# One transpose for the lower columns of two token blocks, and copies within SBUF that double the rows

## What is computed

```python
# mix: w is softmaxed over k, 8 heads of 24 columns share a weight
out = np.einsum('bshk,bskhg->bshg', w, x_unf)
# gated product
gate = 1.0 / (1.0 + np.exp(-(x @ w_gate)))          # 192 -> 1536
y = (gate * (x @ w_val)) @ w_out                    # 1536 -> 192
# rational product
h = y @ w_in                                        # 192 -> 2048
P = a[0] + a[1]*h + a[2]*h**2 + a[3]*h**3
Q = 1.0 + abs(b[0])*abs(h) + abs(b[1])*h**2
z = (P / (Q + 1e-06)) @ w_out2                      # 2048 -> 192
```

## Time and profile before

| | |
|---|---|
| median of 3 runs | 1420.21 us (1420.18 to 1420.8) |
| the profiled execution | 1422.31 us, its span 1420.4 us |
| mean granted clock of PE | 0.993 of full |
| busy share of the span: PE, PEld | 97%, 87% |
| DVE, ACT, POOL | 89%, 76%, 25% |
| mean share of the 16 DMA engines on the SP queue | 7.2% |

### The profile page before, as it was taken

The page is one execution under the profiler, slowest core; times in us unless marked ns, Lnnn a source line. Parts: engine busy times, 40 slices in busy tenths (PEclk is TensorE's granted clock), DMA queues, the critical chain, the costliest instruction groups (busy, mean ns, idle before and its releaser), DMA issues.

```text
span 1420.4 us, 19056 instructions
## 1 busy us (share of the span) xinstructions
PE 1379.2 (97%) x7282; PEld 1238.5 (87%) x7282; DVE 1259.2 (89%) x1504; ACT 1083.4 (76%) x1470; POOL 356.2 (25%) x204
## 2 busy tenths in 40 slices
PE   6899999999999999999999999999999999999976
PEld 5789888888889889889889889889898898889966
DVE  7677989999989989889999989899898898889998
ACT  3387887877777788787787777787787778778975
POOL 0143323231332313233131332323233141210000
PEclk9999999999999999999999999999999999999989
DMA  9100100101010010100101010010100001000000
GB/s 242 59 32 1 38 0 1 42 1 43 1 43 1 1 43 1 43 1 0 43 1 43 0 43 1 0 43 0 42 1 29 11 1 34 1 12 0 12 0 17
DMA packets 13468, 33.06 MB, mean 23 GB/s; under 512 B 1601, under 2 KB 7747, under 8 KB 13377
## 3 DMA queue, kind: packets, MB, share of 16 engines
q1 hardware_dynamic: 13312, 31.85, 7.2%
q0 software_dynamic: 64, 0.00, 0.0%
HBM read 25.55 MB, written 6.29 MB: 22 GB/s over the span
## 4 chain that ended last, share of the span: by engine, by line
PE 90%; DVE 6%; ACT 2%; issue 2%; DMA 0%; SPq 0%; DVEq 0%
PE ring L319 49%; PE acc L346 39%; PE ring L373 1%; PE ring L376 1%; DVE work L712 1%; DVE work L719 1%; DVE work L733 1%; DVE work L706 1%; DVE u L700 1%; DVE work L742 0%; DVE work L726 0%; DVE work L653 0%; DMA window<-in_x_dram 0%; ACT work L485 0%; ACT work L487 0%
## 5 line engine op out<-in xcount | busy, mean ns | idle before, releaser
L346 PE MATMUL acc<-out_w,work 128*128 128x192 f32 x2048 | 366.3, 330 | 14.6 <-DVE work L742 14.6
L346 PEld LDWEIGHTS acc<-out_w,work 128*128 128x128 f32 x2048 | 342.5, 193 | 21.4 <-DVE work L742 15.0
L484 ACT ACTIVATE work<-ring,coef 128x512 f32<-128x512 f32 (+1 forms) x272 | 182.2, 670 | 223.9 <-PE ring L319 221.4
L319 PE MATMUL ring<-yt,in_w 128*128 128x512 f32 (+1 forms) x1360 | 330.8, 389 | 2.4 <-DVE work L712 1.9
L346 PE MATMUL acc<-out_w,u 128*128 128x192 f32 x1536 | 284.8, 327 | 6.3 <-DVE u L700 6.3
L319 PEld LDWEIGHTS ring<-yt,in_w 128*128 128x128 f32 x1360 | 245.7, 189 | 51.4 <-DVE work L712 2.9
L319 PE MATMUL ring<-xt,gate_w 128*128 128x512 f32 (+1 forms) x1020 | 267.5, 392 | 3.4 <-DVE work L712 2.1
L346 PEld LDWEIGHTS acc<-out_w,u 128*128 128x128 f32 x1536 | 256.7, 190 | 13.5 <-DVE u L700 7.2
L319 PE MATMUL ring<-xt,val_w 128*128 128x512 f32 (+1 forms) x1020 | 257.0, 382 | 0.0
L603 POOL TENSOR_TENSOR mixed<-mixed,prod 128x768 f32<-128x768 f32 (+1 forms) x90 | 196.7, 2186 | 169.9 <-DVE u L700 150.7
L598 POOL TENSOR_TENSOR prod<-window,mixw 128x768 f32<-128x768 f32 (+1 forms) x90 | 135.0, 1500 | 408.3 <-DVE work L719 307.1
(11 more groups left out here) (57 smaller groups left out, 921.1 us busy)
## 6 DMA issues: line engine op xcount, KB each, us to landing
window<-in_x_dram SPq DMA_DIRECT2D x14, 960.0 KB, 4.6
out_dram<-zsb SPq DMA_DIRECT2D x15, 384.0 KB, 2.5
out_w<-in_moe_w_out_dram SPq DMA_DIRECT2D x1, 1536.0 KB, 19.1
mixw<-in_weight_gen_dram SPq DMA_DIRECT2D x13, 112.0 KB, 2.9
out_w<-in_moe_w_out_dram SPq DMA_DIRECT2D x2, 576.0 KB, 8.7
work<-in_moe_w_in_dram SPq DMA_DIRECT2D x2, 512.0 KB
work<-in_moe_w_in_dram SPq DMA_DIRECT2D x4, 256.0 KB, 13.4
window<-in_x_dram SPq DMA_DIRECT2D x1, 768.0 KB, 4.3
```

What stands on the lines that cost most here:

```text
L319: last = nc.tensor.matmul(dst, wt[:, c], xs[:, 0:n], start=at == 0, stop=at == 4)
L346: last = nc.tensor.matmul(dst, src[:, n * P:(n + 1) * P], w[:, i, :], start=i == 0 and n % 2 == 0, stop=i == last_i and n % 2 == 1, skip_g ...
L484: nc.scalar.activation(den(n), h, ACT.Abs, scale=coef[:, 6:7])
```

## The change

For x tiles from the third on and for all y tiles, the lower columns of two neighbouring token blocks stand side by side in one block of 128 columns (`x_side`, `y_side`), and one transpose turns both: the rows 0 to 63 that come out belong to the first block, rows 64 to 127 to the second. ACT and DVE split this half-as-wide bank into `xs[0]`, `xs[1]` (or `ys`), and SP issues copies from SBUF to SBUF that put each half of the rows into both halves of `xt[..][2]` and `[3]` (or `yt`): four transfers for the high part as soon as ACT has written it, four for the low part when DVE has. PE's first product of the tile waits for all eight. `x_twice` is left for the first two tiles only; POOL writes the last add of a mix in two instructions, the second straight into `x_side`.

```diff
+            def spread(part, n, dst, signal):
+                for h in range(2):
+                    src = part[h * DB:(h + 1) * DB, 0:n * P // 2].rearrange("p (a t) -> p a t", t=P)
+                    for d in range(2):
+                        to = dst[d * DB:(d + 1) * DB, 0:n * P].rearrange("p (a h t) -> p a h t", h=2, t=P)
+                        sp.dma_start(to[:, :, h, :].bitcast(F32), src.bitcast(F32)).then_inc(signal, 16)
+            def spread_x(j):
+                sp.wait_ge(s_xh, 2 * j + 2)
+                spread(xs[0], BLOCKS[j], xt[j % 2][2], s_xs)
+                sp.wait_ge(s_x, 2 * j + 2)
+                spread(xs[1], BLOCKS[j], xt[j % 2][3], s_xs)
...
             for c in range(EARLY, NCH):
                 if c + 1 < NCH:
                     load_weights(c + 1)
+                if c >= 3:
+                    spread_y(c - 3)
                 load_window(c)
                 if c >= 4:
                     store(c - 4)
+                if c > EARLY:
+                    spread_x(c - 1)
...
                 if i == 0:
                     pe.wait_ge(s_x, 2 * j + 2)
+                    wait(pe, s_xs, 128 * (j - EARLY + 1))
...
                 if i == 0:
                     pe.wait_ge(s_y, 2 * j + 2)
+                    pe.wait_ge(s_ys, 128 * (j + 1))
...
-                for n in range(BLOCKS[j]):
+                for n in range(count):
                     last = nc.tensor.transpose(bank(u, j, 1)[:, n * P:(n + 1) * P], lower(n), ident[:, :])
...
+                    pe.wait_ge(s_mix, MIXES * (j - EARLY + 1))
+                    transposes("X", j, lambda n: mixed[:, n, 0:DA],
+                               lambda n: x_side[:, n * P:(n + 1) * P], BLOCKS[j] // 2).then_inc(s_xT, 1)
...
+                nc.scalar.copy(xs[0][:, 0:n // 2], bank("X", j, 1)[:, 0:n // 2]).then_inc(s_xh, 1)
...
-                nc.scalar.copy(dst[:, :, :, 0:D], src)
-                nc.scalar.copy(dst[:, :, :, D:2 * P], src[:, :, :, DA:D]).then_inc(s_ysb, 1)
+                nc.scalar.copy(ysb[:, 0:n * DA].rearrange("p (a n d) -> p a n d", n=2, d=DA), src[:, :, :, 0:DA])
+                nc.scalar.copy(y_side[:, 0:n * DB].rearrange("p (a n d) -> p a n d", n=2, d=DB),
+                               src[:, :, :, DA:D]).then_inc(s_ysb, 1)
...
-                if k % 4 == 3 and k > 3:
-                    x_twice(k // 4 + 1)
...
+                if k == MIXES - 1:
+                    nc.gpsimd.tensor_tensor(mixed[:, 0:n, 0:DA], mixed[:, 0:n, 0:DA], prod[:, 0:n, 0:DA], ALU.add)
+                    nc.gpsimd.tensor_tensor(x_side[:, 0:n * DB].rearrange("p (n d) -> p n d", d=DB), mixed[:, 0:n, DA:D],
+                                            prod[:, 0:n, DA:D], ALU.add).then_inc(s_mix, 1)
+                    return
...
+                nc.vector.tensor_tensor(xs[1][:, 0:n // 2], bank("X", j, 1)[:, 0:n // 2],
+                                        xs[0][:, 0:n // 2].bitcast(F32), ALU.subtract).then_inc(s_x, 1)
```

More of the change, by code:

```diff
@@ L116, in moe_kernel @@
         yt = [[sb(f"yt{b}_{n}", [P, T], F32R) for n in range(4)] for b in range(2)]
-        x_pair = sb("x_pair", [P, J, 2, DB])
-        ysb = sb("ysb", [P, J, 2 * P])
+        xs = [sb(f"xs{n}", [P, T // 2], F32R) for n in range(2)]
+        ys = [sb(f"ys{n}", [P, T // 2], F32R) for n in range(2)]
+        x_side = sb("x_side", [P, J * 2 * DB])
+        ysb = sb("ysb", [P, J * DA])
+        y_side = sb("y_side", [P, J * DB])
         zsb = sb("zsb", [P, J, D])
@@ L191, in moe_kernel @@
         s_x = sem("x_ready")
+        s_xs = sem("x_lower_rows_spread")
         s_gate = sem("gate_done")
@@ L200, in moe_kernel @@
         s_y = sem("y_ready")
+        s_ys = sem("y_lower_rows_spread")
         s_h = sem("h_done")
@@ L282, in load_weights, with spread_y @@
                 sp.dma_start(weights(c), wg_rows[:, OFFS[c] * HK:OFFS[c + 1] * HK]).then_inc(s_weights[c % FIRST], 16)
+            def spread(part, n, dst, signal):
[9 more added lines that the diff above has]
+                spread(xs[1], BLOCKS[j], xt[j % 2][3], s_xs)
+            def spread_y(j):
+                sp.wait_ge(s_yh, 2 * j + 2)
+                spread(ys[0], BLOCKS[j], yt[j % 2][2], s_ys)
+                sp.wait_ge(s_y, 2 * j + 2)
+                spread(ys[1], BLOCKS[j], yt[j % 2][3], s_ys)
             def store(j):
@@ L308, in _ @@
                     store(c - 4)
-            for j in range(NCH - 4, NCH):
+                if c > EARLY:
+                    spread_x(c - 1)
+            spread_y(NCH - 3)
+            store(NCH - 4)
+            spread_x(NCH - 1)
+            spread_y(NCH - 2)
+            store(NCH - 3)
+            spread_y(NCH - 1)
+            for j in range(NCH - 2, NCH):
                 store(j)
@@ L367, in out2, with transposes @@
                 second_product(acc2, out2_w, num(n), i, F2 - 1, BLOCKS[j]).then_inc(s_out2, 1)
-            def transposes(u, j, upper, lower):
+            def transposes(u, j, upper, lower, count):
                 wait_bank(pe, u, j, 0)
@@ L379, in x_transposes @@
             def x_transposes(j):
-                pe.wait_ge(s_twice, j + 1)
-                transposes("X", j, lambda n: mixed[:, n, 0:DA],
-                           lambda n: x_pair[:, n, :, :].rearrange("p a d -> p (a d)")).then_inc(s_xT, 1)
+                if j < EARLY:
+                    pe.wait_ge(s_twice, j + 1)
+                    transposes("X", j, lambda n: mixed[:, n, 0:DA],
+                               lambda n: x_side[:, n * P:(n + 1) * P], BLOCKS[j]).then_inc(s_xT, 1)
+                else:
+                    pe.wait_ge(s_mix, MIXES * (j - EARLY + 1))
+                    transposes("X", j, lambda n: mixed[:, n, 0:DA],
+                               lambda n: x_side[:, n * P:(n + 1) * P], BLOCKS[j] // 2).then_inc(s_xT, 1)
             def y_transposes(j):
                 pe.wait_ge(s_ysb, j + 1)
-                transposes("Y", j, lambda n: ysb[:, n, 0:DA], lambda n: ysb[:, n, DA:2 * P]).then_inc(s_yT, 1)
+                transposes("Y", j, lambda n: ysb[:, n * P:(n + 1) * P], lambda n: y_side[:, n * P:(n + 1) * P],
+                            BLOCKS[j] // 2).then_inc(s_yT, 1)
             def keep_busy(count, m=0):
@@ L441, in x_twice @@
             def x_twice(j):
[L442 to L447, removed]
+                act.wait_ge(s_early, EARLY_STEPS * OFFS[j + 1])
                 wait(act, s_xT, j)
                 n = BLOCKS[j]
-                nc.scalar.copy(x_pair[:, 0:n, :, :], mixed[:, 0:n, DA:D].unsqueeze(2).to_broadcast([P, n, 2, DB])
+                nc.scalar.copy(x_side[:, 0:n * 2 * DB].rearrange("p (n a d) -> p n a d", a=2, d=DB), mixed[:, 0:n, DA:D].unsqueeze(2).to_broadcast([P, n, 2, DB])
                                ).then_inc(s_twice, 1)
@@ L459, in x_high @@
                 nc.scalar.copy(dst[0][:, 0:n], bank("X", j, 0)).then_inc(s_xh, 1)
-                nc.scalar.copy(dst[2][:, 0:n], bank("X", j, 1)).then_inc(s_xh, 1)
+                if j < EARLY:
+                    nc.scalar.copy(dst[2][:, 0:n], bank("X", j, 1)).then_inc(s_xh, 1)
+                    return
+                wait(act, s_xs, 128 * (j - EARLY))
+                nc.scalar.copy(xs[0][:, 0:n // 2], bank("X", j, 1)[:, 0:n // 2]).then_inc(s_xh, 1)
             def y_high(j):
@@ L468, in y_high @@
                 nc.scalar.copy(dst[0][:, 0:n], bank("Y", j, 0)).then_inc(s_yh, 1)
-                nc.scalar.copy(dst[2][:, 0:n], bank("Y", j, 1)).then_inc(s_yh, 1)
+                wait(act, s_ys, 128 * j)
+                nc.scalar.copy(ys[0][:, 0:n // 2], bank("Y", j, 1)[:, 0:n // 2]).then_inc(s_yh, 1)
             def sigmoid(m):
@@ L680, in x_low @@
                 dve.wait_ge(s_xh, 2 * j + 2)
-                nc.vector.tensor_tensor(dst[3][:, 0:n], bank("X", j, 1), dst[2][:, 0:n].bitcast(F32),
-                                        ALU.subtract).then_inc(s_x, 1)
+                if j < EARLY:
+                    nc.vector.tensor_tensor(dst[3][:, 0:n], bank("X", j, 1), dst[2][:, 0:n].bitcast(F32),
+                                            ALU.subtract).then_inc(s_x, 1)
+                    return
+                nc.vector.tensor_tensor(xs[1][:, 0:n // 2], bank("X", j, 1)[:, 0:n // 2],
+                                        xs[0][:, 0:n // 2].bitcast(F32), ALU.subtract).then_inc(s_x, 1)
             def y_low(j):
@@ L691, in y_low @@
                 dve.wait_ge(s_yh, 2 * j + 2)
-                nc.vector.tensor_tensor(dst[3][:, 0:n], bank("Y", j, 1), dst[2][:, 0:n].bitcast(F32),
-                                        ALU.subtract).then_inc(s_y, 1)
+                nc.vector.tensor_tensor(ys[1][:, 0:n // 2], bank("Y", j, 1)[:, 0:n // 2],
+                                        ys[0][:, 0:n // 2].bitcast(F32), ALU.subtract).then_inc(s_y, 1)
             def gated(m):
```

2 lines of the change are left out of this document (1 added, 1 removed).

## The result

The changed kernel takes 1412.99 us (median of 5 runs, 1410.86 to 1413.46) against 1420.8 us of the kernel before beside it (5 runs, 1420.18 to 1422.01): ratio 0.9942, 95% interval 0.9927 to 0.9956. The forecast was 1413.8 us in a range of 1411.2 to 1418.6. The profiled execution took 1412.99 us with a span of 1411.1 us.

The account below looks back on a forecast made before the run. PE, busy throughout 130 to 1320 us, was taken to bound the kernel. 59 transposes x 0.109 = 6.4 us, all else counted at nothing: 1420.2 - 6.4 = 1413.8 us, range 1411.2 to 1418.6 us.

Parts of the forecast that it names:

- What bounds the kernel: From 130 to 1320 us PE is busy 1190.00 of 1190.00 us; time off DVE or ACT gains nothing there.
- The price of a transpose: On PE, one lower transpose removed saves 0.109 us, the distance from start to start, not its 273 ns busy time.
- Rival D: On PE, each removed transpose gives back its busy time, 59 x 0.273 = 16.1 us, so 1404 us; chance 2%.
- 59 of 61: Of 61 transposes removed, 59 lie where PE sets the time, 6.4 us; first and last y tile's count at nothing.
- Can the others follow: DVE and ACT keep up when quarters with x transposes shorten from 21.59 to 21.37 us; a 20.70 us quarter showed no wait.
- rival C: Shorter quarters end in PE waits on DVE's bank releases; half or more of the gain goes, 1417 to 1420 us; 7%.
- The copies: Eight SBUF copies per tile, 0.5 us per issue and 2.9 us to landing, arrive before PE's first product, 4 us to spare.
- The budget: Time from ready rows to PE's first product: 10.9 us for x, 15.7 for y, 7.9 at the third x tile.
- rival A: Slower copies come 1.6 us late at the first pass of each of 15 x tiles, 24 us: 1438 us; 6%.
- Rival B: Each tile's eight copies run strictly one after another with own landings, 20 us, late for x and y: 1615 us; 3%.
- The last y tile: In the tail PE waits some 2.3 us more for copies, ahead of its wait for DVE's quotient; counted at nothing.
- Either way: Half-clock pieces in the tail may shift: 1.3 us at the end, about as much earlier, 2.6 us to either side.

Follow-up runs that it names:

- fillers: Products of the identity, results unused, put ahead of six PE waits for DVE: 1412.69 us in the changed kernel, 1418.86 us in the kernel before.

## Why the prediction was right

**What bounds the kernel.** Right, and shown: with the transposes put back the time is that of before, although ACT and DVE then have less to do. Time off them alone is worth nothing in this stretch.

**The price of a transpose.** 0.109 us from the distance of starts, 0.111 by the lead that grew over 57 of them. Rival D, with the busy time of 273 ns, is out: the rows of after still show 273 ns, and the gain is not 16 us.

**59 of 61.** Both that I counted at nothing lie where PE waits for DVE. The trace cannot tell 0.1 us there from other shifts; it is not shown one by one.

**Can the others follow.** Yes; the list of PE's waits from 130 to 1310 us is empty, so rival C is out.

**The copies.** I took 0.5 us per issue and 2.9 us to landing; measured are 0.65 and, for most copies, 2.0. The two errors nearly cancel, and that was luck: 4 us to spare forecast, 3.2 found in the tile shown and 4.3 at the median landing; at the third x tile 1.0 forecast, 1.2 found. The budget as a point of decision is shown by the copies in halves, which turn the gain into a loss. SP's issue time is the larger part of the chain: 4.5 us pass until the last copy is issued. One sign of being wrong that I had named did come, issues on SP above 1 us (up to 1.41 us for an x copy, 1.65 for a y copy, 1.48 for the load behind the x copies), and PE waited for none of them. My worst issue of the start was misread as well: the view of the earlier trace rows has a pair of 2.08 us at 18.03, so rival A's far end is 8 x 1.04 + 4.6 = 12.9 us, not 12.5.

Rival B, each copy behind the landing of the one ahead, is out: eight copies whose landings take 2.0 to 3.1 us were all done 7.7 us after the first issue, not after 16. The sentence of the Trainium skill that I held against the change, in "DMA: Bandwidth & Descriptors", section "Rules for kernel authors", says that two transfers to disjoint partition halves serialize, and gives as its reason that both use the same DMA engines. Only my reading of it as one landing after the other is refuted; whether the data of the copies share the engines' time, no run here shows. The 2 us of fixed cost stand on that page of the Trainium skill, in "Anatomy of one DMA", for transfers that GpSimd issues; the copies here are issued by SP, and 2.0 us is their median all the same.

**POOL.** I took 2.2 us for its two adds; they take 1.24 + 1.66 = 2.9 us on average, inside the bounds of 1.82 and 3.64. Covered, as worked out: PE waits for neither from 130 to 1310 us.

**The last y tile.** A wait of 2.3 us forecast, 1.6 listed (1.9 by the distance of starts, as with the copies in halves). It costs nothing that can be measured, nor does the like wait put into the kernel before.

**The size.** 6.4 us forecast, 7.8 in the record, and the interval of its ratio (6.2 to 10.4 us) holds 6.4 and 6.6 alike. The traces fix what the transposes give far better than whole runs do: 6.35 us from the third x tile to the sixteenth y tile, in both executions of the changed kernel. What comes on top lies ahead of this stretch and behind it, where one kernel differs from itself. "Either way" was the right word for the tail, but its 2.6 us were too few: by the earlier trace rows the earlier slow piece is 5.49 - 2 x 1.47 = 2.55 us, not about 1.3. In the profiled execution the tail gave 2.7 us more, and 2 of the 10 runs of the changed kernel lie below 1411.2; that the median fell inside the range is in this part luck.

That the tail came out faster by the change's own wait was my first theory afterwards, and it fell. Without fillers the runs do go with the granted clock (the changed kernel at 0.998 near 1410.8 us, at 0.994 near 1414.6), but it is not all a matter of the clock, since runs of the kernel before with fillers, at 0.999, still lie 2.4 us apart (1417.22 to 1419.65). Whether the change makes the tail faster stays open. From the sixteenth y tile on it took 113.8 and 113.9 us in the profiled executions without fillers and without the change (the kernel before, and with a wait added), and 111.0 to 112.2 in the six that hold the change or a part of it, the one with the transposes put back among them. But those two lie near the upper end of their kernels' runs (1422.31 and 1422.15 us), and with fillers in both kernels the tails differ by 0.2 us.

## What to carry to other kernels

Where one engine shows no idle time for a long stretch, price an instruction on it by the distance from start to start, and count work on other engines at nothing; putting the removed work back as a dummy, with everything else of the change left in, is the experiment that proves it. Compare such a stretch between the same two instructions of two traces: here it repeated to 0.02 us, while whole runs of one kernel lay 4 to 6 us apart. Copies within SBUF can take over a rearrangement from a busy PE if their whole time, issues included, fits between the last split and the first use: count the issues, since sixteen instead of eight turned a gain of 7 us into a loss of 8.

## What the runs showed that I had not expected

- A copy of 64 KB occupied SP for 0.65 us from start to start, more than a load of 112 KB (0.43 us), and a copy of half the bytes for about the same: 16 in 10.52 us.
- The load of the mixing weights right behind the x copies shown held SP for 1.48 us instead of 0.43 (0.59 is the median over the kernel), and a store's landing took 3.6 us instead of 2.5.
- POOL's add of 256 columns took 1.66 us on average, that of 512 columns ahead of it 1.24 us.
